# The prologue of an attention-and-MLP kernel: loads in another order, first scores in memory of their own, decays and masks in halves

## The reference

```python
for t in range(S):
    kt, vt, rt = (k[:, :, t], v[:, :, t], r[:, :, t])
    cur = np.einsum('bhd,bhe->bhde', u[None] * kt, vt)
    y[:, :, t] = np.einsum('bhd,bhde->bhe', rt, state + cur)
    state = w[None, :, :, None] * state + np.einsum('bhd,bhe->bhde', kt, vt)
```

## Time and profile before

| | |
|---|---|
| median of the timed runs | 864.17 us |
| the profiled execution, its time | 864.71 us |
| its span, first to last instruction | 863.2 us |
| TensorE matmuls busy | 856.6 us, 99% |
| VectorE, ScalarE, GpSimd busy | 499.6, 378.0, 177.2 us |
| granted TensorE clock | 1.000 |

### The profile page before, as it was taken

How to read it: one execution, slowest core, us unless ns; L and a number is a source line. 1 busy time by engine, 2 the same in 40 slices (tenths; PEclk the granted TensorE clock), 3 DMA queues, 4 the chain that set the end, 5 groups by cost and what they waited for, 6 DMA issues and landing times.

```text
span 863.2 us, 14254 instructions
## 1 busy us (share of the span) xinstructions
PE 856.6 (99%) x6253; PEld 709.3 (82%) x6253; DVE 499.6 (58%) x558; ACT 378.0 (44%) x398; POOL 177.2 (21%) x116
## 2 busy tenths in 40 slices
PE   8999999999999999999999999999999999999998
PEld 7888888788888888888888888888888888888886
DVE  7797766655666665554369554554554554454443
ACT  5687766556666556666697221121121120220211
POOL 4673334332333442200236200000000000000000
PEclk9999999999999999999999999999999999999999
DMA  7554331222123112102223110110110000100101
GB/s 277 205 155 159 108 136 60 63 89 63 54 83 125 59 63 89 64 2 83 82 83 120 65 36 1 37 36 1 37 37 1 36 1 1 37 0 1 38 1 36
DMA packets 19777, 56.62 MB, mean 66 GB/s; under 512 B 2944, under 2 KB 5248, under 8 KB 19712
## 3 DMA queue, kind: packets, MB, share of 16 engines
q1 hardware_dynamic: 14688, 44.87, 15.7%
q10 hardware_dynamic: 5024, 10.82, 3.5%
HBM read 44.28 MB, written 9.44 MB: 62 GB/s over the span
## 4 chain that ended last, share of the span: by engine, by line
PE 97%; DVE 1%; DMA 1%; issue 0%; POOL 0%; ACT 0%; DVEq 0%; POOLq 0%
PE y_ps L870 45%; PE h_ps L813 34%; PE a_ps L813 11%; PE a_ps L674 2%; PE a_ps L651 1%; PE a_ps L664 1%; PE y_ps L681 1%; DMA tables<-in_u 0%; DMA mid<-in_w 0%; PE a_ps L705 0%; PE y_ps L705 0%; PE h_ps L694 0%; PE a_ps L718 0%; PE a_ps L723 0%; DVE mid L1094 0%
## 5 line engine op out<-in xcount | busy, mean ns | idle before, releaser
L813 PE MATMUL h_ps<-x_split,win_hi 128*128 128x512 f32 (+1 forms) x864 | 265.9, 389 | 0.9 <-issue 0.8
L870 PE MATMUL y_ps<-g_hi,wout_hi 128*128 128x512 f32 x576 | 224.2, 389 | 0.0
L870 PE MATMUL y_ps<-g_lo,wout_hi 128*128 128x512 f32 x576 | 224.1, 389 | 0.0
L870 PE MATMUL y_ps<-g_hi,wout_lo 128*128 128x512 f32 x576 | 224.0, 389 | 0.0
L813 PEld LDWEIGHTS h_ps<-x_split,win_hi 128*128 128x128 f32 x864 | 159.8, 188 | 34.3 <-issue 1.2
L813 PE MATMUL h_ps<-x_split,win_lo 128*128 128x512 f32 (+1 forms) x432 | 166.8, 386 | 0.0
L1223 DVE TENSOR_TENSOR g_lo<-mid,g_hi 128x1024 fp32r<-128x1024 f32 x96 | 150.2, 1564 | 3.3
L1230 DVE TENSOR_TENSOR mid<-mid 128x1024 f32<-128x1024 f32 x48 | 61.0, 1271 | 143.4 <-ACT mid L988 143.4
L870 PEld LDWEIGHTS y_ps<-g_hi,wout_hi 128*128 128x128 f32 x576 | 108.1, 188 | 22.9 <-DVE g_lo L1223 0.4
L870 PEld LDWEIGHTS y_ps<-g_hi,wout_lo 128*128 128x128 f32 x576 | 108.1, 188 | 22.4
L870 PEld LDWEIGHTS y_ps<-g_lo,wout_hi 128*128 128x128 f32 x576 | 108.1, 188 | 22.4
(11 more groups left out here) (135 smaller groups left out, 811.8 us busy)
## 6 DMA issues: line engine op xcount, KB each, us to landing
att<-in_att SPq DMA_DIRECT2D x20, 584.0 KB, 5.9
att<-in_att SPq DMA_DIRECT2D x20, 512.0 KB, 3.6
w_raw<-in_w_in SPq DMA_DIRECT2D x16, 384.0 KB, 3.1
w_raw<-in_w_out SPq DMA_DIRECT2D x16, 384.0 KB, 3.1
x_dram<-mid ACTq DMA_DIRECT2D x6, 768.0 KB, 3.3
att<-x_dram SPq DMA_DIRECT2D x6, 768.0 KB, 4.5
out<-mid ACTq DMA_DIRECT2D x5, 768.0 KB, 3.8
mid<-in_first_T SPq DMA_DIRECT2D x2, 512.0 KB, 4.5
```

The costliest lines, as they stand in the source:

```text
L813: m = nc.tensor.matmul(ps, a, b_, start=n == 0, stop=n == len(terms) - 1)
L870: m = nc.tensor.matmul(y_ps[:, o, :], a, b_, start=unit == 0 and t == 0 and j == 0, stop=unit == UNITS - 1 and t == 1 and j == 2, skip_gro ...
```

## The change

w stays first on SyncE's queue, and on ScalarE's u_cols now goes ahead of T of item 0. SyncE's loads behind them are ordered anew: n of item 0 before the wait for mid_free, weight block 0 behind T of items 2 and 3, the other n between v and weights, u right behind them without a wait. The four first items get score memory of their own, which lies where g_hi and g_lo lie later; the fillers read a part of win_lo instead of g_hi. Waits that guarded shared score memory go. GpSimd clears all_scores at its start. VectorE's product of item 0 stands in the last level of the table and that of item 1 behind the table; decays of items 0 and 1 and masks of items 0 and 1 are each done in two halves (decays by head pairs, masks by the two head sides), and TensorE waits for the halves. TensorE has 5, 7 and 2 fillers in place of 9, 5 and 3, the transposes of the k table ahead of the own sums of item 1, and the own sums of item 2 behind main part 1. ScalarE's first_x_hi of items 0 and 1 stand ahead of weight_hi 0, its k_pow ahead of weight_hi 1. VectorE's weight_lo 2 stands behind mask_scores of item 4. A hunk that only puts slow_sum in the place of first_sum is left out here.

```diff
--- before.py
+++ after.py
@@ -86,2 +86,9 @@
 
+
+        with ExitStack() as until_units:
+            first_memory = [until_units.enter_context(nc.sbuf_tensor(f"first_scores{i}", [128, H * ITEM], f32))
+                            for i in range(PER)]
+        g_hi = [sb(f"g_hi{i}", [128, 2, GROUP], f32r) for i in range(2)]
+        g_lo = [sb(f"g_lo{i}", [128, 2, GROUP], f32r) for i in range(2)]
+
         win_hi, win_lo = sb("win_hi", [128, KT, DFF], f32r), sb("win_lo", [128, KT, DFF], f32r)
@@ -92,4 +99,2 @@
         mid = sb("mid", [128, 4 * 1024 + KT * GROUP])
-        g_hi = [sb(f"g_hi{i}", [128, 2, GROUP], f32r) for i in range(2)]
-        g_lo = [sb(f"g_lo{i}", [128, 2, GROUP], f32r) for i in range(2)]
         att = [sb(f"att{i}", [128, A_COLS]) for i in range(2)]
@@ -120,7 +125,5 @@
         slow_sum = tables[:, 2 * DM:2 * DM + 2 * ITEM].rearrange("p (i t) -> p i t", t=ITEM)
-        first_sum = kr_product[0][:, 0:2 * ITEM].rearrange("p (i t) -> p i t", t=ITEM)
         scores = [all_scores[:, i] for i in range(2)]
-        first_scores = [tables[:, :].rearrange("p (s a t) -> p s a t", s=2, t=ITEM),
-                        all_scores[:, :, :, :, :].rearrange("p i s a t -> p (i s a t)")
-                        .rearrange("p (s a t) -> p s a t", s=2, t=ITEM)]
+        first_scores = [t[:, :].rearrange("p (s a t) -> p s a t", s=2, t=ITEM) for t in first_memory]
+        idle = win_lo[:, 0, DFF - GROUP:]
         k_powT, r_powT = pow_kr[:, 0], pow_kr[:, 1]
@@ -247,3 +250,3 @@
         x2_hi_done, x2_done = sem("x2_hi_done"), sem("x2_done")
-        last_halves, sum_zeroed = sem("last_halves"), sem("sum_zeroed")
+        last_halves, scores_half = sem("last_halves"), sem("scores_half")
 
@@ -351,6 +354,5 @@
             load_first_T(1)
-            load_weights(0)
             load_first_v(0)
             load_first_v(1)
-            load_weights(1)
+            load_first_n(0)
             sp.wait_ge(mid_free, 1)
@@ -358,6 +360,10 @@
             load_first_T(3)
+            load_weights(0)
+            load_first_n(1)
             load_first_v(2)
             load_first_v(3)
-            for n in range(PER):
-                load_first_n(n)
+            load_weights(1)
+            load_first_n(2)
+            load_first_n(3)
+            sp.dma_start(u_all, u.partition_broadcast(128)).then_inc(u_in, 16)
             load_weights(2)
@@ -365,4 +371,2 @@
             load_chunk(5)
-            sp.wait_ge(first_out_ps, 3)
-            sp.dma_start(u_all, u.partition_broadcast(128)).then_inc(u_in, 16)
             for j in range(3, len(W1_FIRST) + W_BUFS - 1):
@@ -400,3 +404,3 @@
         def _(pool):
-            pool.memset(g_hi[0][:, 0, :].bitcast(f32), 0.0).then_inc(idle_zeros, 1)
+            pool.memset(idle.bitcast(f32), 0.0).then_inc(idle_zeros, 1)
             pool.memset(ident, 0.0).then_inc(zeroed, 1)
@@ -412,2 +416,3 @@
             pool.memset(state[:, :], 0.0).then_inc(state_zeroed, 1)
+            pool.memset(all_scores[:, :, :, :, :], 0.0).then_inc(masks, 1)
 
@@ -482,15 +486,12 @@
                 if n == 1:
-                    pool.wait_ge(early_T, 2)
-                else:
-                    pool.wait_ge(first_out_ps, n - 1)
+                    pool.wait_ge(early_T, 4)
                 sums = own[:, 1, :].rearrange("p (a s) -> p s a", s=2)
                 for hh in range(2):
-                    m = pool.affine_select(out=first_scores[1][:, hh, :, :],
-                                           in_=sums[:, hh, :].unsqueeze(2).to_broadcast([128, PAIRS, ITEM]),
-                                           compare_op=ALU.is_equal, fill=0.0, base=0, pattern=[[0, PAIRS], [-1, ITEM]],
-                                           channel_multiplier=1)
-                m.then_inc(odd_diag, 1)
+                    pool.affine_select(out=first_scores[n][:, hh, :, :],
+                                       in_=sums[:, hh, :].unsqueeze(2).to_broadcast([128, PAIRS, ITEM]),
+                                       compare_op=ALU.is_equal, fill=0.0, base=0, pattern=[[0, PAIRS], [-1, ITEM]],
+                                       channel_multiplier=1).then_inc(odd_diag, 1)
 
             def first_product(n):
-                pool.wait_ge(early_T, n)
+                pool.wait_ge(early_T, 2 * n)
                 pool.wait_ge(t_in[n], 16)
@@ -602,3 +603,3 @@
                 if slow:
-                    pool.memset(first_sum, 0.0).then_inc(slow_x, 1)
+                    pool.memset(slow_sum, 0.0).then_inc(slow_x, 1)
                     pool.wait_ge(slow_x, 1)
@@ -607,7 +608,3 @@
                 multiply_kr(PER)
-                pool.wait_ge(first_out_ps, PER)
-                pool.memset(all_scores[:, :, :, :, :], 0.0).then_inc(masks, 1)
                 if slow:
-                    pool.memset(slow_sum, 0.0).then_inc(sum_zeroed, 1)
-                    pool.wait_ge(sum_zeroed, 1)
                     release(0, 1)
@@ -638,3 +635,3 @@
                 for _ in range(count):
-                    nc.tensor.matmul(h_ps[:, 1, :], g_hi[0][:, 0, 0:128], g_hi[0][:, 0, :], start=True, stop=True)
+                    nc.tensor.matmul(h_ps[:, 1, :], idle[:, 0:128], idle, start=True, stop=True)
 
@@ -698,3 +695,2 @@
             def first_item_scores(n):
-                pe.wait_ge(early_T, n + 1)
                 if n >= 2:
@@ -703,2 +699,4 @@
                 for p in range(PAIRS):
+                    if p % 2 == 0:
+                        pe.wait_ge(early_T, 2 * n + 1 + p // 2)
                     for hh in range(2):
@@ -712,9 +710,12 @@
                 pe.wait_ge(n_in[n], 16)
-                pe.wait_ge(scores_done, n + 1)
                 bank = work_banks(n)[:, 0, :]
-                for a in range(KT):
+                for a in (0, 2, 1):
                     q, hh = divmod(a, 2)
+                    if a == 0 and n < 2:
+                        pe.wait_ge(scores_half, n + 1)
+                    elif a == 0 or hh == 1:
+                        pe.wait_ge(scores_done, n + 1)
                     for i in range(2):
                         nc.tensor.matmul(bank[side(i), a * ITEM:(a + 1) * ITEM], first_slot(n, a, i),
-                                         first_scores[n % 2][:, hh, 2 * q + i, :], start=a == 0, stop=False,
+                                         first_scores[n][:, hh, 2 * q + i, :], start=a == 0, stop=False,
                                          skip_group_check=True)
@@ -723,3 +724,3 @@
                         m = nc.tensor.matmul(bank[i * PAD + 2 * GAP:(i + 1) * PAD, a * ITEM:(a + 1) * ITEM],
-                                             first_piece(n, a, i), first_scores[n % 2][:, 1, 2 + i, :], start=False, stop=True,
+                                             first_piece(n, a, i), first_scores[n][:, 1, 2 + i, :], start=False, stop=True,
                                              skip_group_check=True)
@@ -881,3 +882,3 @@
             pe.wait_ge(idle_zeros, 1)
-            keep_warm(9)
+            keep_warm(5)
             pe.wait_ge(consts, 4)
@@ -885,8 +886,5 @@
             nc.tensor.matmul(extra_bank[0:1, 0:1], inside_min, ones, start=True, stop=True).then_inc(count_ps, 1)
-            keep_warm(5)
+            keep_warm(7)
             first_own(0)
-            keep_warm(3)
-            first_own(1)
-            first_item_scores(0)
-            first_item_scores(1)
+            keep_warm(2)
 
@@ -896,4 +894,6 @@
             m.then_inc(k_table_ps, 1)
+            first_own(1)
+            first_item_scores(0)
+            first_item_scores(1)
             first_main(0)
-            first_own(2)
 
@@ -904,2 +904,3 @@
             first_main(1)
+            first_own(2)
             first_states(0)
@@ -927,4 +928,4 @@
         def _(act):
+            act.dma_start(u_side[:, :, :], u_cols).then_inc(u_side_in, 16)
             act.dma_start(buf(0)[:, 0:T_COLS], first_T[0]).then_inc(t_in[0], 16)
-            act.dma_start(u_side[:, :, :], u_cols).then_inc(u_side_in, 16)
             act.wait_ge(consts, 4)
@@ -938,3 +939,3 @@
                 if n == 3:
-                    act.wait_ge(odd_diag, 1)
+                    act.wait_ge(odd_diag, 2)
                 act.activation(own[:, n % 2, :], h_ps[:, 0, 0:H], ACT.Copy).then_inc(own_done, 1)
@@ -944,6 +945,4 @@
                 act.wait_ge(own_done, n + 1)
-                if n >= 2:
-                    act.wait_ge(first_out_ps, n - 1)
                 for p in range(PAIRS):
-                    m = act.activation(first_scores[n % 2][:, hh, p, :], ident, ACT.Copy,
+                    m = act.activation(first_scores[n][:, hh, p, :], ident, ACT.Copy,
                                        scale=own[:, n % 2, 2 * p + hh:2 * p + hh + 1])
@@ -1031,9 +1030,12 @@
             m.then_inc(k_wide_done, 1)
+            first_x_hi(0)
+            first_x_hi(1)
             weight_hi(0)
-            first_x_hi(0)
             first_own(2)
             first_fill(2, 0)
-            first_x_hi(1)
             first_fill(2, 1)
```

(48 more changed lines are left out.)

## The result

The changed kernel took **866.75 us** (median of 20 runs, 864.77 to 872.94), the kernel before 864.25 beside it (20 runs, 863.27 to 866.43). The ratio is **1.0036, with a 95% interval of 1.002 to 1.0052**: slower, by 0.2 to 0.5%, where 862.1 was forecast. The profiled execution of after took 865.12 us, 0.41 more than that of before, so it is one of the quick ones of its kernel; most of the loss of the median, 2.5 us, is in executions which it doesn't show.

The account below looks back on a forecast made before the run. TensorE was taken as the bound, rigid after 39 us, so prologue savings last. 4.9 - S + 0.45 + 0.2 = 2.05 us for S = 3.5, and 864.17 - 2.05 = 862.1 us; range 861.2 to 863.6.

Parts of the forecast that it names:

- (a): Prologue load of w, now ahead of ScalarE's large load: lands 2.45 us after issue instead of 3.40, bounds 1.9 and 3.40.
- (d): Scores to main part 0: two sets take 2.28 us, halved decays and masks keep up, main part 0 at S+8.73.
- (e): Main part 0 to first dense product: reordered work and loads covered, priced at nothing, 0.3 us if cover is gone.
- (c): TensorE up to first scores: own sums 0 from S+3.4, two fillers 0.5 us, first scores at S+6.45.
- rival (3): Fewer fillers and pauses leave TensorE's clock low from first scores through main part 1: slower, 868 us; chance 0.05.
- Rival (1): GpSimd's clearing holds VectorE's first table step until 4.25: gain only 1.3 us, 862.9; chance 0.32.
- S: Moment when w has landed and VectorE starts its table of powers: 4.46 before, 3.5 forecast.
- The choice of 0: Price of GpSimd's clearing beside VectorE's first table step: taken as 0, up to 0.75 us possible.
- G: How much sooner TensorE starts main part 0: 4.9 - S, 1.4 us for S = 3.5.
- (f): Early u and no all_scores waits remove the gap before item 4: 0.45 us; weight_lo 1 ends about 0.2 us ahead.
- (g): Unit 1's second product, block at 53.88, waits for g_lo: 0.2 us of 0.29 taken back, bounds 0 and 0.29.

Follow-up runs that it names:

- run 3: The kernel before with fillers 5, 7 and 2 in place of 9, 5 and 3, all else as it was: 870.76 us, ratio 1.0078.
- the second profile: The changed kernel again, nothing edited, for a second trace (span 868.5 us) and set of times: 870.02 us, ratio 1.0049.
- run 2: The changed kernel with the fillers of before, 9, 5 and 3 in place of 5, 7 and 2: 865.15 us, ratio 0.9999.
- run 4: The changed kernel with GpSimd's clearing of all_scores moved from its start to behind mid_free, fillers 5, 7 and 2: 867.21 us, ratio 1.0025.
- run 11: The kernel before with only ScalarE's first loads reordered, u_cols ahead of T0: 867.48 us, ratio 1.0023.
- run 6: The kernel before with one filler fewer in the third group, 9, 5 and 2: 866.82 us, ratio 1.0018.
- run 12: The kernel before with own memory for first scores, all_scores cleared at the start, u early, mask 4 ahead of weight_lo 2: 864.04 us, ratio 0.9993.
- run 7: The changed kernel with GpSimd's split of weight block 0 behind decay 3 and fillers 9, 5 and 3: 864.96 us, ratio 1.0001.
- run 8: The changed kernel with GpSimd's split of weight block 0 behind decay 3, the clearing behind mid_free, fillers 7, 6 and 3: 865.5 us, ratio 0.9997.

## Why the prediction was wrong

**The view of what bounds the kernel held in the main.** Between the two profiles of after, 4.7 of 4.9 us arise ahead of the first block of unit 2; but breaks behind it come and go too, the largest 2.63 us (run 3). And "TensorE is busy" isn't "TensorE is at full speed": the prologue can lose nearly 5 us with no wait to show for it.

**The loss in parts.** The first profile of after has a span of 863.6 instead of the 861.2 forecast. Of these 2.4 us 0.99 are lost up to main part 0 (parts (a) to (d)), 0.87 behind it (e) and 0.55 in a break, 0.22 come back near 170, and 0.2 are small pieces. The other 2 us of the median are the level.

**The step that failed is (c), with rival (3).** It priced the fillers by time alone, two at 0.25 us "as TensorE is warm by then", and took the three fewer as neutral. Measured: the seven behind the count matmul took 3.29 us, 0.47 each, the two took 0.58, and own sums 0 started at 8.30 where product 0 was ready at 7.64 (6.96 + 0.68 on VectorE). Rival (3) had the mechanism, roughly the place (it took the level to fall at the first scores, where in the second profile it hadn't risen before them) and nearly the price (868; the second profile gives 870.04), and a chance of 0.05. Its facts were there, fewer fillers and a pause of TensorE near 4; the pause near 6.6 wasn't, as the seven slow fillers filled it. What the text missed is that the level needn't be low in each execution to move the median: of after's 20 runs ten took over 867 us, of the 20 of before beside them none. It took the one profiled execution of before, with the level up by 6.9 us, for the rule. Runs 2 and 3 show from both sides that the fillers are the cause; that it works by the level is read from the durations in the profiles, and why it stays down so long behind a pause of half a microsecond stays open.

**Rival (1), given 0.32, came true as well.** The clearing held the first step to 4.23. The price is slightly less than taken: the second step starts at 4.26, which answers to an S of 4.05 (before it came 0.21 behind the first, 4.67 after 4.46), not 4.25. From there VectorE kept the forecast: table's end 8.42 (S + 4.4 = 8.45), decays from 9.10 (S + 5.0 = 9.05). The choice of 0 was wrong in its reason: neither four columns nor a clearing that reads nothing protects. The Trainium skill, SBUF — State Buffer, section "Who interferes with whom", says that a VectorE step in a two-port mode and a GpSimd instruction exclude each other, and that whoever issues first has the shared ports for the whole instruction. The trace agrees on the exclusion, with 1.46 us for a step that takes 0.17. It doesn't bear out the order: by the recorded starts the step (2.77) came ahead of the clearing of all_scores (3.25), and was held to that clearing's end all the same.

**(a) was mis-sized the other way.** w took 1.70 us, less than the lower bound of 1.9 and well under the 2.45 chosen; runs 4 and 11 confirm it (first step at 2.77 and 2.81). But the 3.40 that it was compared with is one execution: in the four profiles with the old order w took 3.4, 2.8, 2.7 and 3.0 us (before, runs 3, 6 and 12), in the ten with the new one 1.7 to 2.0. The new order shortens the load, by 0.7 to 1.7 us. T0 then sets the pace, as the part said: in run 4 VectorE waited 0.43 us for it, in run 11 2.17.

**(d)** From own sums 0 to the first scores 2.83 us were measured (8.30 to 11.13; 3.05 forecast), and two sets of scores took 2.09 (2.28 forecast). The halved decays and masks kept up. G was 0.41 instead of 1.4: 0.55 lost to S (4.05 for 3.5), 0.85 to own sums 0 (8.30 where S + 3.4 is 7.45), and 0.22 and 0.19 won back by these two pieces.

**(e) was priced at nothing and cost 0.87 us.** From main part 0 to the first product of unit 0 it took 9.69 us instead of 8.82. The cover, that scores 3 have decay 3 "0.7 us in time", went because decay 3 itself took 1.0 us longer beside GpSimd's split of weight block 0; by the chain scores 3 waited 0.35 and took 1.16 instead of 0.89, and main part 0 took 0.16 more. The text knew this kind of collision from weight_lo 2 and looked for it in two places, not here. In runs 7 and 8 decay 3 takes 1.21 us. By the same page and section of the Trainium skill, a VectorE step with two inputs in SBUF collides with a GpSimd instruction that reads SBUF, and not with one that only writes it. The split reads SBUF, and the trace agrees: decay 3 ends 1.1 us behind the split, about its own length.

**(f) and (g) were right.** 0.45 and 0.27 us went, as forecast (0.45, and 0.2 of at most 0.29). The thin cover in (f) held, with weight_lo 1 at 1.50 us.

**What was not foreseen and stays open:** the break of 0.55 at 68.14, which eats (f) or (g). Such breaks without a cause come and go: 1.08 us near 73 in the second profile of after, 1.22 and 0.61 in run 4, 2.63 near 42 in run 3, none in run 12. No run tests them.

## What to carry to other kernels

Matmuls that only keep TensorE at its level are a part of the timing: look for pauses of the engine behind them, change their number and place last, one at a time, and judge by many executions, for one profile shows only one outcome. Read the duration of a known matmul through the prologue (here 16 score matmuls, 1.16 or 2.08 us), not only busy shares and the mean clock. When an operation moves on GpSimd, look at every VectorE step that will now run beside it, small ones too.

## What the runs showed of the hardware that was not expected

- The level fell back to 1.2 GHz while TensorE was busy 5.00 of 5.00 us, for up to 20 us (run 6). The Trainium skill, TensorE: Matmul & The Clock Gate, "HAM oscillation — how this bites in real kernels", ties such a fall to pauses in which TensorE waits for a DMA; here the list of TensorE's waits names none in that stretch. Ends of matmuls are modelled, so short pauses between small ones could lie hidden in the 5.00; no run here shows them.
- The mean granted clock doesn't count the first stretch at the lower level: 1.000 stands beside a trace in which it lasts to 19.6 us. Later falls are in it (0.988 in run 6).
- The first stretch at the lower level lasted to some 6.9 us in before. In after, with the same instructions, it lasted to between 8.3 and 9.2 us in one profile and to 19.6 in the other; in run 3 it lasted to between 16.9 and 17.9. These three are the profiles with a pause of 0.53 to 0.72 us behind TensorE's first 2.5 us of work; in the other eleven it had ended before 8.
- Two GpSimd memsets, one behind the other, held a VectorE step of four columns until the second had ended (0.17 us became 1.46), though the second started after the step; one memset alone made it 0.56 (run 4). A split that reads SBUF made a decay of 1.22 us last 2.24.
- A load of 2 KB landed in 1.7 to 2.0 us where the large load on the other queue was issued later (ten profiles), and in 2.7 to 3.4 where it was issued right beside it (four).
